# A recurrent attention stage with three products taken off TensorE: mask, carry, and a bank for each bias half

## What is computed

```python
for t in range(S):
    m_new = np.maximum(f_gate[:, :, t] + m, i_gate[:, :, t])
    f_stab = np.exp(f_gate[:, :, t] + m - m_new)
    i_stab = np.exp(i_gate[:, :, t] - m_new)
    m = m_new
    C = f_stab[..., None, None] * C + i_stab[..., None, None] * np.einsum('bhd,bhe->bhde', vt, kt)
    n = f_stab[..., None] * n + i_stab[..., None] * kt
    h_tilde = np.einsum('bhde,bhe->bhd', C, qt)
    denom = np.maximum(np.abs(np.einsum('bhd,bhd->bh', n, qt)[..., None]), 1.0)
    y[:, :, t] = sigmoid(o_gate[:, :, t]) * h_tilde / denom
```

## Time and profile before

| what | us |
|---|---|
| median of 3 runs (range) | 909.55 (909.12 to 910.09) |
| the profiled execution by itself | 914.29 |
| its span, first to last instruction | 912.5 |
| PE busy in the span | 849.8 (93%) |
| DVE, ACT, POOL busy in the span | 509.3, 394.0, 110.7 |
| mean granted TensorE clock | 0.964 |

### The profile page before, as it was taken

One profiled execution on the slowest core, in us unless ns is written; L12 is line 12 of the kernel. 1 busy time (PEld: TensorE's weight loads), 2 busy tenths in 40 slices (PEclk: granted clock), 3 DMA queues, 4 the chain that ended last, 5 costly groups with the idle time before them and its releaser, 6 DMA issues.

```text
span 912.5 us, 18039 instructions
## 1 busy us (share of the span) xinstructions
PE 849.8 (93%) x6301; PEld 743.1 (81%) x6301; DVE 509.3 (56%) x1060; ACT 394.0 (43%) x714; POOL 110.7 (12%) x151
## 2 busy tenths in 40 slices
PE   5999999915999999999994999999999999999997
PEld 2777777615999999999993788888888888888886
DVE  4466566555788787878772344354354354453432
ACT  4444444404777767677761232232232233233122
POOL 4234454340000000000001100100100100100000
PEclk8899999966999999999997999999999999999999
DMA  6354445258889999999961100100100100100000
GB/s 166 89 146 129 147 140 165 72 200 279 251 266 262 266 269 279 264 253 291 296 203 37 30 1 1 58 1 1 58 0 0 58 0 0 58 0 2 28 1 29
DMA packets 76567, 109.37 MB, mean 120 GB/s; under 512 B 11380, under 2 KB 55284, under 8 KB 76516
## 3 DMA queue, kind: packets, MB, share of 16 engines
q1 hardware_dynamic: 72036, 98.20, 36.7%
q0 software_dynamic: 2304, 7.88, 2.6%
q10 hardware_dynamic: 2176, 2.62, 0.9%
HBM read 92.21 MB, written 16.47 MB: 119 GB/s over the span
## 4 chain that ended last, share of the span: by engine, by line
PE 85%; issue 5%; DMA 3%; ACT 2%; POOL 2%; DVE 1%; ACTq 1%; SPq 1%; POOLq 0%; DVEq 0%
PE psum L1419 42%; PE psum L1494 5%; PE psum L1495 5%; PE psum L1496 5%; PE psum L1443 4%; PE psum L1445 4%; PE psum L1444 4%; PE psum L1279 3%; PE psum L1330 2%; PE psum L1353 2%; PE psum L1306 2%; PE psum L1298 2%; PE psum L1299 1%; DMA w_raw<-w 1%; PE psum L1411 1%
## 5 line engine op out<-in xcount | busy, mean ns | idle before, releaser
L1242 DVE TENSOR_TENSOR gated_lo<-gated,gated_hi 128x512 fp32r<-128x512 f32 x72 | 49.9, 693 | 185.7 <-ACT gated_hi L807 185.7
L802 ACT ACTIVATE sigm_sb<-psum 128x512 f32<-128x512 f32 x72 | 43.0, 598 | 255.8 <-PE psum L1419 255.8
L1419 PE MATMUL psum<-nT_hi,w_gv_hi 128*128 128x512 f32 x432 | 125.1, 398 | 2.6 <-DVE nT_lo L1229 2.6
L1419 PE MATMUL psum<-nT_lo,w_gv_hi 128*128 128x512 f32 x432 | 124.5, 396 | 0.0
L1419 PEld LDWEIGHTS psum<-nT_lo,w_gv_hi 128*128 128x128 f32 x432 | 81.5, 189 | 19.9
L1419 PEld LDWEIGHTS psum<-nT_hi,w_gv_hi 128*128 128x128 f32 x432 | 79.0, 189 | 16.9 <-DVE nT_lo L1229 2.8
L1419 PE MATMUL psum<-nT_hi,w_gv_lo 128*128 128x512 f32 x288 | 90.6, 396 | 0.0
L635 POOL DMA_INDIRECT c_rows<-y_by_slot,slot_idx x24 | 22.8, 948 | 555.8 <-DMA y_by_slot<-y_tile 286.3
L1494 PE MATMUL psum<-w_out_hi,gated_hi 128*128 128x320 f32 x288 | 89.8, 312 | 0.0
L1495 PE MATMUL psum<-w_out_lo,gated_hi 128*128 128x320 f32 x288 | 89.1, 309 | 0.0
L1496 PE MATMUL psum<-w_out_hi,gated_lo 128*128 128x320 f32 x288 | 89.0, 309 | 0.0
(11 more groups left out here) (222 smaller groups left out, 1571.5 us busy)
## 6 DMA issues: line engine op xcount, KB each, us to landing
w_raw<-w SPq DMA_DIRECT2D x38, 640.0 KB, 6.9
w_raw<-w SPq DMA_DIRECT2D x38, 512.0 KB, 4.5
w_raw<-w SPq DMA_DIRECT2D x76, 128.0 KB, 5.1
kv_tok<-tok SPq DMA_DIRECT2D x24, 324.0 KB, 4.4
qk_sb<-qk SPq DMA_DIRECT2D x48, 160.0 KB
y_by_slot<-y_tile SPq DMA_DIRECT2D x12, 321.0 KB, 7.3
og_tok<-o_tok SPq DMA_DIRECT2D x24, 160.0 KB, 2.2
x_tile<-x_by_expert SPq DMA_DIRECT2D x12, 320.0 KB, 2.9
```

Source lines behind the costliest of these rows:

```text
L802: nc.scalar.activation(sigm_sb[f % 2][:], bank[2 * (f % 2)][:], ACT.Sigmoid).then_inc(sig_ready, 1)
L1242: dve.tensor_tensor(gated_lo[f % 4][:], gated[f % 2][:], gated_hi[f % 4][:].bitcast(F32), ALU.subtract).then_inc(hv_lo, 1)
L1419: m = mm(dst, w, x, start=(n == 0), stop=(n == len(terms) - 1))
```

## The change

- The mask is no longer added to the bias. After `probs`, POOL sets the entries of `prob_T` above the diagonal to zero by an `affine_select` of 128x512 fp32 for each half (`mask(n, h)`), and the value part of `attend` waits for these (`probs_masked`). `maskT` and its identity are gone; TensorE's warming products use a cleared tile `warm16`, made early by DVE.
- The carry weights are no longer split into two parts and spread by a product. ACT's exponential writes them straight into the row store, and SP broadcasts them from DRAM into an SBUF tile `carry[b]`, two DMAs per chunk (64 and 40 partitions, four rows of 512 B each). `carried` (DVE) and `fade` (POOL) read this tile; ACT's `decay` copy is gone.
- The bias halves have banks 0 and 1 of their own and are made one behind the other, before the scores. The gates use bank 1, one chunk further ahead (`gate_turn(i+3)`, four gate buffers), and their loads are a DMA step of their own on SP (`gate_load`).
- At the start the select rows are built from a small `select` tile by ACT copies, three gate turns stand ahead of `front(0)`, and SP's order is changed: second `rows_store` and `group_rows` before the router loads.

```diff
-        CARRY, BIAS, SCORES, OUT_T, OUT, STATE = bank[0], bank[1], bank[2:4], psum[:, 4:6], bank[6], bank[7]
+        BIAS, SCORES, OUT_T, OUT, STATE = bank[0:2], bank[2:4], psum[:, 4:6], bank[6], bank[7]
...
+            def gate_load(n):
+                c, b = divmod(n, B)
+                i = b * NC + c
+                wait(sp, og_ready, n - B + 1)
+                sp.dma_start(og_tok[b][:, 0:DM], o_tok[i * P:(i + 1) * P, :]).then_inc(og_in[b], 16)
+
+            def carry_rows(n):
+                c, b = divmod(n, B)
+                wait(sp, qa_ready, n - 2 * B + 1)
+                wait(sp, state_faded, n - 2 * B + 1)
+                for r in range(2):
+                    w = 64 if r == 0 else D
+                    sp.dma_start(carry[b][64 * r:64 * r + w],
+                                 row_dram[c, 4, b * H:(b + 1) * H].rearrange("(a r) t -> r a t", r=2)[r].partition_broadcast(w)).then_inc(carry_in[b], 16)
...
+            gate_load(0)
             loads(0)
+            gate_load(1)
+            gate_load(2)
             loads(1)
             rows_store(0)
             group_rows(0)
-            query_rows(0)
-            query_rows(1)
+            for n in range(B):
+                query_rows(n)
             loads(2)
             loads(3)
-            query_rows(2)
-            query_rows(3)
             rows_store(1)
+            gate_load(3)
+            group_rows(1)
...
-            group_rows(1)
             for n in range(B, NT):
+                carry_rows(n)
                 loads(n)
                 query_rows(n)
+                if n < NT:
+                    gate_load(n)
...
+            def mask(n, h):
+                pool.wait_ge(probs_ready, 2 * n + h + 1)
+                t = prob_T[n % 2][:, h]
+                pool.affine_select(out=t, in_=t, compare_op=ALU.is_ge, fill=0.0, base=0,
+                                   pattern=[[0, HH], [1, P]], channel_multiplier=-1).then_inc(probs_masked, 1)
...
             def fade(n):
-                pool.wait_ge(decay_ready, n - B + 1)
+                pool.wait_ge(carry_in[b], 32 * c)
...
-                                   decay[n % 2][q].unsqueeze(2).to_broadcast([64 + D, HP, D1]), ALU.mult).then_inc(state_faded, 1)
+                                   carry[b][q, :, P - 1:P].to_broadcast([64 + D, HP, D1]), ALU.mult).then_inc(state_faded, 1)
...
+            mask(0, 0)
             weigh(0)
+            mask(0, 1)
             constants()
             for i in range(NT + 1):
                 if i >= 1:
                     gated_heads(i - 1)
                 if B <= i < NT - B:
                     fade(i)
+                if i + 1 < NT:
+                    mask(i + 1, 0)
                 if i + 1 < NT - B:
                     weigh(i + 1)
+                if i + 1 < NT:
+                    mask(i + 1, 1)
                 if i >= 2 * B:
                     scatter(i - 2 * B)
...
+            act.wait_ge(select_made, 1)
+            selected(0)
             rows_high(0)
             act.wait_ge(gate_rows_made, 1)
             gates(0)
-            act.wait_ge(select_made, 1)
-            for b in range(1, B):
-                nc.scalar.activation(bias_query[b][0:2 * H], bias_query[0][0:2 * H].bitcast(F32), ACT.Copy).then_inc(select_copied, 1)
+            selected(1)
+            gates(1)
+            selected(2)
+            gates(2)
             rows_high(1)
             for h in range(2):
                 weights(0, h)
-            gates(1)
+            selected(3)
...
-                dve.wait_ge(carry_ready, n - B + 1)
+                dve.wait_ge(carry_in[b], 32 * c)
...
-                                  CARRY[q], ALU.mult).then_inc(qa_ready, 1)
+                                  carry[b][q].rearrange("p a t -> p (a t)"), ALU.mult).then_inc(qa_ready, 1)
...
-                wait(pe, weights_ready, 2 * n)
+                wait(pe, weights_ready, 2 * n - 2 if n >= 3 else 0)
+                wait(pe, tanh_ready, n)
...
-                if c:
-                    wait(pe, qa_ready, n - B)
-                    wait(pe, decay_ready, min(n - B, NT - 2 * B))
-                    mm(CARRY, parity[:], bias_carry[p][:, b * HP:(b + 1) * HP].rearrange("r a t -> r (a t)"), start=True, stop=True).then_inc(carry_ready, 1)
-                pe.wait_ge(tanh_ready, n + 1)
                 for h in range(2):
+                    wait(pe, weights_ready, 2 * n - 1 + h)
                     if h:
-                        pe.wait_ge(weights_ready, 2 * n + 1)
-                    mm(BIAS, bias_key[p][:, b], bias_query[b][:].rearrange("r (a q) t -> r q a t", q=2)[:, h], start=True, stop=False)
-                    mm(BIAS, ident16[:], maskT[:].rearrange("p a t -> p (a t)"), start=False, stop=True).then_inc(bias_ready, 1)
...
+                        pe.wait_ge(tanh_ready, min(max(n + 2, 3), NT))
+                    mm(BIAS[h], bias_key[p][:, b], bias_query[b][:].rearrange("r (a q) t -> r q a t", q=2)[:, h], start=True, stop=True).then_inc(bias_ready, 1)
...
-                pe.wait_ge(probs_ready, 2 * n + 2)
+                pe.wait_ge(probs_masked, 2 * n + 2)
...
+            keep_warm(6)
             pe.wait_ge(ident_made, 1)
-            gate_turn(0)
-            keep_warm(14)
-            pe.wait_ge(mask_made, 3)
-            pe.wait_ge(select_copied, B - 1)
+            for n in range(3):
+                gate_turn(n)
+                keep_warm(2)
             front(0)
-            gate_turn(1)
...
-                if i + 2 < NT:
-                    gate_turn(i + 2)
+                if i + 3 < NT:
+                    gate_turn(i + 3)
```

More of the change, by code:

```diff
@@ L138, in build @@
         gate_half = sb("gate_half", [P, 2], F32, ga)
-        gate = [sb(f"gate{i}", [P, HH * P], F32, ga) for i in range(3)]
+        gate = [sb(f"gate{i}", [P, HH * P], F32, ga) for i in range(4)]
         oT = [sb(f"oT{i}", [P, 2, 2 * P], F32, ga) for i in range(2)]
@@ L157, in build @@
         bias_query = [sb(f"bias_query{b}", [18, H, P], F32R, ga) for b in range(B)]
-        bias_carry = [sb(f"bias_carry{i}", [4, B * HP, P], F32R, ga) for i in range(2)]
+        carry = [sb(f"carry{b}", [P, HP, P], F32, ga) for b in range(B)]
+        select = sb("select", [2 * H, H], F32, ga)
         row_i = sb("row_i", [BH, NC, P], F32, ga)
@@ L161, in build @@
         row_ones = sb("row_ones", [BH, P], F32, ga)
[L162 removed]
+        parts = [sb(f"parts{i}", [BH, 5, P], F32R, ga) for i in range(2)]
         row_fsum = sb("row_fsum", [BH, P], F32, ga)
@@ L215, in build @@
         key_in = [sem(f"key_in{i}") for i in range(2)]
-        carry_in = [sem(f"carry_in{i}") for i in range(2)]
+        carry_in = [sem(f"carry_in{b}") for b in range(B)]
         query_in = [sem(f"query_in{b}") for b in range(B)]
@@ L538, in _ @@
             pool.tensor_tensor(gate_rows[:], gate_half[:, 0:1], gate_half[:, 1:2], ALU.add).then_inc(gate_rows_made, 1)
[L539 to L547, removed]
+            mark(pool.memset(head_out[:], 0.0))
+            mark(pool.memset(tri[:], 1.0))
+            settle()
             to_heads = head_out[:, :, :, 0:D]
@@ L647, in rows_high @@
                 act.wait_ge(rows_scanned, c + 1)
-                g_hi, g_lo, mu_hi, mu_lo, a_hi, a_lo = (parts[c % 2][:, n] for n in range(6))
+                g_hi, g_lo, mu_hi, mu_lo = (parts[c % 2][:, n] for n in range(4))
                 nc.scalar.activation(g_hi, row_g[:], ACT.Copy).then_inc(row_high, 1)
@@ L849, in rows_scan @@
             def rows_scan(c):
-                wait(dve, row_high, 2 + 3 * (c - 1) if c else 0)
+                wait(dve, row_high, 2 * c)
+                wait(dve, row_exp, c - 1)
                 wait(dve, rows_out, 16 * (c - 1))
@@ L861, in rows_low @@
             def rows_low(c):
-                dve.wait_ge(row_high, 2 + 3 * c)
-                g_hi, g_lo, mu_hi, mu_lo, a_hi, a_lo = (parts[c % 2][:, n] for n in range(6))
+                dve.wait_ge(row_high, 2 * c + 2)
+                g_hi, g_lo, mu_hi, mu_lo = (parts[c % 2][:, n] for n in range(4))
                 dve.tensor_tensor(g_lo, row_g[:], g_hi.bitcast(F32), ALU.subtract).then_inc(rows_ready, 1)
@@ L866, in rows_low, with carried @@
                                          op0=ALU.mult, op1=ALU.subtract).then_inc(rows_ready, 1)
-                if c:
-                    dve.tensor_tensor(a_lo, row_a[:], a_hi.bitcast(F32), ALU.subtract).then_inc(rows_ready, 1)
-            def carry(n):
-                b = n % B
-                dve.wait_ge(qk_in[b], 32 * (n // B) + 32)
-                dve.wait_ge(carry_ready, n - B + 1)
+            def carried(n):
+                c, b = divmod(n, B)
+                dve.wait_ge(qk_in[b], 32 * c + 32)
+                dve.wait_ge(carry_in[b], 32 * c)
                 wait(dve, chunk_done, n - 1)
@@ L994, in _ @@
                 if B <= i + 1 < NT:
-                    carry(i + 1)
+                    carried(i + 1)
                 if i >= 2:
```

98 lines of the change are left out of this document (34 added, 64 removed).

## The result

The changed kernel takes 969.66 us (median of 4 runs, 966.05 to 973.32), the kernel before 909.82 (909.12 to 911.25): the ratio is 1.0656, 95% interval 1.061 to 1.0702. It is slower by 60 us where 27 us less were forecast, and outside the range.

What follows compares the result with a forecast made beforehand. PE, busy 130.63 of 130.99 us in the steady stretch, was taken as the bound. Gains of 9.9 (start), 16.7 (steady) and 0.8 (tail), 27.4 us, gave 882 us from 909.55; forecast 876 to 888, range 873 to 895.

Steps and rivals of the forecast that it cites:

- the DMA paragraph: Steady periods: two broadcasts a chunk make DMA busy 5.2 of 5.97 us, tight, but loads come two periods ahead; no cost.
- Banks, gates, decay: Steady periods: the moved bias products wait for nothing, and ACT's lost decay copy gains nothing; no cost.
- 2 to 3 us late, of 12: Group-row chunks: SP stands 3.9 us for the row store, so the next chunk's loads come late; counted as nothing.
- The one on the other side: Rival, chance 0.05: broadcasts make DMA the bound from 163 ns a descriptor; at 200 ns the kernel takes 929 us.
- The rival of POOL and DVE in each other's way: Rival, chance 0.22: selects near 1.11 us and zT held behind carried() make periods 6.1 to 6.45, total 890 us.
- upside of 0.10: Steady periods: the second bias product, directly behind another, may shrink from 0.43 to 0.33 us; left out of the sum.
- The charge of 1.5 us for DVE and POOL: Steady periods: choose() beside POOL's selects delays carried(), which meets zT; 0.3 us charged for 5 of them.
- The start: Before the first c = 1 period: front(0) has data at 12.5, that period begins at 34.0 instead of 43.91; gain 9.9 us.
- the case that had been held at 35: Start: if the clock drops to 1.2 GHz as before, chunk 0 costs some 4 us more and hides the router wait.
- The tail: Last chunks: without two masks and the carry, head columns of chunk 22 follow at 6.85 instead of 7.61 us; gain 0.76.
- the steady periods: 19 chunk periods: carry and two mask products leave PE, 6.93 to 5.97 us each; 18.2 minus 1.5 gives 16.7 us.
- The rule of the Trainium skill that the prediction cites: A DVE operation with two SBUF inputs and a GpSimd operation reading SBUF exclude each other for a whole instruction.

Runs made afterwards that it cites:

- e4: Changed kernel with each output-gate load still issued after the attention of chunk n - 4, but first of that chunk's loads instead of last: 900.15 us, ratio 0.9862.
- e1: Changed kernel with each output-gate load issued by SP one chunk earlier, nothing else changed: 887.96 us, ratio 0.971 to the kernel before.
- e3: Kernel before the change, with only its gate loads from chunk 4 on issued one chunk later, behind the next chunk's loads: 947.77 us, ratio 1.0399.
- e8: e1 with the broadcast of the carry rows done twice per chunk, into a second tile nobody reads: 916.68 us, ratio 1.0055 to the kernel before.
- e7: e1 with each select on POOL done twice, the extra one into a tile nobody reads: 905.47 us, ratio 0.9921 to the kernel before.
- e6: e1 with the mask back on PE as two products per chunk and no selects on POOL: 898.93 us, ratio 0.9865 to the kernel before.
- e5: e1 plus 7, 4 and 8 warming products in three waits of PE at the start: 888.18 us, ratio 0.9742 to the kernel before.

## Why the prediction was wrong

**The step that failed** is in the DMA paragraph: "each load of chunk n is issued two periods (12 us) before its reader". It is true of qk, kv and query rows. For the gate load the diff did two things at once, and I costed neither: its reader moved one chunk ahead (`gate_turn(i+3)`), and its issue moved behind `loads(n)`, which holds SP until the attention of chunk n - 4 has ended. I looked at the load's own wait (`og_ready`, long met) and not at what SP stands on before it. Its lead is the 3.37 us from the end of that attention to the gate turn, less 1.5 us of issues, against 2.2 to 4.1 us of landing. Under "Banks, gates, decay" I checked the waits of the two bias products, for exponentials and tanh; the gate turn's wait for `og_in` I did not. The late chunk behind the row store was seen there too and called nothing, "2 to 3 us late, of 12": e4 shows a wait of 2.04 us in it. It was no term of the sum at all; it measured 0.095 of the old time, some 86 us (the changed kernel against e1), and in e3 4% by itself.

**The rivals** missed it too. The one on the other side put the loss on the DMA engines' time per descriptor. In the changed kernel they are busy 0.39 of the steady stretch and in e1 0.69 of 5.9 us, 4.1 us, where the prediction had 5.2. By that the change adds about 0.8 us, an estimate of 30 ns a descriptor instead of 74; by e8, which doubles the broadcasts (0.73 of 7.4 us, 5.4 us), it is 1.4 us, or 53 ns. In the changed kernel a transfer was late, and the engines were not full in the mean. The rival of POOL and DVE in each other's way does not show in e1's steady periods; its mechanism shows in e7, with twice the selects.

**What held**, shown by e1, in which only this step is mended: selects 0.63 us (0.70 forecast), zT at 0.81 to 2.07 (0.80 to 2.06), qa 0.69, period 5.87 with the shrink of the second bias product that was named as an upside of 0.10 (5.97), no wait for carry or qk. From 39.71 to the last chunk the 19 periods take 111.8 us, 19.2 less than before against 16.7 forecast. The charge of 1.5 us for DVE and POOL was of the right kind: mu_lo, next to the selects, takes 0.56 us in the mean of six in e1, and 0.27 in e6, which has no selects, and it costs PE little: the 19 periods are 0.9 us longer in all than 18.2 and the upside of 19 x 0.10 would make them.

**The start** gave 4.2 us in e1 (39.71 against 43.91), not 9.9. The row store was issued at 6.09 as forecast, but bias_key followed only at 11.6, so landing took 5.5 us and not 3.9, and front(0) started another 2.3 us later, at 13.94 (the prediction took about 2 for the small loads, without a row for it); the clock fell at 17.3, the case that had been held at 35, and chunks 0 and 1 ran at 1.2 GHz until 34.5. The gate load is in this too: PE waited 1.63 us before 21.70 for the one issued at 16.22. e5 shows the part of the clock: 3.0 us.

**The tail** did not give 0.8 us but cost 1.3. From the last period to the end of the attention stage e1 takes 18.2 us, 16.9 before: head columns of chunk 22 follow at 7.27 us, not 6.85, and behind two waits of 2.0 us for zT PE is at 1.2 GHz (the last head columns take 2.06 us, 1.15 before).

**Sum of e1 in the prediction's own terms:** 4.2 + 19.2 - 1.3 + 2.6 = 24.7 us of span (912.5 to 887.8), against 27.4. The last term came behind the attention stage, which I had let shift as a block. So the total is near the forecast partly by luck: the steady periods, the main term, were right in mechanism and size, while the start gave less than half. e1 at 0.971 beats both kernels, and no other run here is shown to be faster.

## What to carry to other kernels

When a diff moves a load or its reader, write down for each load the event that its queue stands on when it comes to it, and the time from that event to the reader; compare with issue plus landing. The instruction's own wait tells nothing if the one ahead of it in the queue waits for something later. And price a wait of PE of 2 us in a period of 6 at more than 2 us: here the clock that fell after it cost at least two thirds as much again (at least some 35 us beside at most 51).

## What the runs showed of the hardware

- **The clock falls at waits that leave PE mostly busy.** In the changed kernel PE is busy for 165 of 186 us and the mean clock is 0.66; eight waits of 1.9 to 3.4 us, in periods of 8.1 to 11.5, bring it to 1.2 GHz each time. In the profiled execution of e3, with waits of 0.5 to 1.4 us in most periods, of 7.5 to 8.4, it stays at 0.98, with two falls, behind waits of 2.05 and 0.86 us; its other executions have lower clocks. In e7 it fell behind a wait of 0.71. So the length of one wait does not tell. The Trainium skill (TensorE: Matmul & The Clock Gate, section "HAM oscillation — how this bites in real kernels") describes such an alternation with longer waits for DMA; here waits from 1.9 us up did it.
- **A DVE operation with two SBUF inputs can be held by several POOL operations in a row.** In e7 it took 1.96 us instead of 0.19, until three POOL instructions in a chain had ended, and 1.97 us once more. The rule of the Trainium skill that the prediction cites speaks of one instruction.
- **A 128x512 bf16 product behind a bias product costs 0.42 us, not 0.32,** since the product before it gets 0.1 longer (e6).
- **Landing depends on what is queued ahead.** The same 160 KB gate load took 2.2 us (before) and 2.4 (e4) as the first of a chunk's loads, 4.1 (changed kernel) and 5.0 (e1, where it does no harm) as the last; medians.
- The later signal of e5 (0.38 us instead of 0.12 behind an unchanged sequence) is open; e1 has it too, 0.50 us, in its first two periods.
